# Placing the attention stages of a fused linear-attention and two-MoE kernel: scores one step later, decay and q scaling behind the hidden-layer work

## The reference

```python
for t in range(S):
    state = alpha[:, :, t, :, None] * state + np.einsum('bhd,bhe->bhde', k[:, :, t], v[:, :, t])
    y[:, :, t] = np.einsum('bhd,bhde->bhe', q[:, :, t], state)
# x = y as (B * S, H * D)
h = x @ w_in
x = (np.maximum(h, 0.0) + alpha * np.minimum(h, 0.0)) @ w_out
h = x @ w_in2
g = np.where(h >= 1, h, np.where(h <= -1, 0.0, (h + 1) ** 2 / 4))
y = g @ w_out2
```

## Time and profile before

| | us |
|---|---|
| median of 3 runs | 977.68 |
| lowest and highest | 975.34 and 981.53 |
| the profiled execution | 981.99 |
| its span | 980.3 |
| PE busy in it | 946.6 |
| DVE busy | 448.1 |
| ACT busy | 302.8 |
| POOL busy | 354.8 |
| mean granted clock of PE, share of full | 0.977 |

### The profile page before, as it was taken

How to read it: one execution, slowest core, us unless ns; L and a number is a source line. 1 busy time by engine, 2 the same in 40 slices (tenths; PEclk the granted TensorE clock), 3 DMA queues, 4 the chain that set the end, 5 groups by cost and what they waited for, 6 DMA issues and landing times.

```text
span 980.3 us, 13041 instructions
## 1 busy us (share of the span) xinstructions
PE 946.6 (97%) x5050; PEld 815.9 (83%) x5050; DVE 448.1 (46%) x732; ACT 302.8 (31%) x561; POOL 354.8 (36%) x322
## 2 busy tenths in 40 slices
PE   7888999899999999999999999999999999999998
PEld 6877999889988888888888888888888888888886
DVE  4566546656555554455532444333333333333332
ACT  2323222222322232232224543233233332332322
POOL 5234333323223232222324764434334334343332
PEclk8777999999999999999999999999999999999999
DMA  5721113111311111112011320010010010100101
GB/s 162 212 46 33 33 34 63 35 33 33 65 33 33 33 33 33 33 37 49 13 65 32 97 66 1 1 33 1 1 33 1 0 33 1 33 1 1 32 1 33
DMA packets 21101, 37.02 MB, mean 38 GB/s; under 512 B 2160, under 2 KB 14448, under 8 KB 21040
## 3 DMA queue, kind: packets, MB, share of 16 engines
q1 hardware_dynamic: 21040, 36.19, 15.7%
HBM read 31.47 MB, written 4.72 MB: 37 GB/s over the span
## 4 chain that ended last, share of the span: by engine, by line
issue 43%; PE 32%; POOL 20%; DVE 3%; DMA 1%; SPq 0%; ACT 0%; POOLq 0%; DVEq 0%; ACTq 0%
POOL g_lo L303 16%; PE h_ps L670 4%; PE y_ps L670 4%; PE y_ps L672 4%; PE y_ps L671 4%; PE h_ps L672 4%; PE h_ps L671 4%; PE a_ps L640 2%; POOL x_lo L310 2%; POOL w_lo L283 2%; PE a_ps L616 1%; PE a_ps L636 1%; PE a_ps L628 1%; DVE prod L467 1%; DVE inv L474 1%
## 5 line engine op out<-in xcount | busy, mean ns | idle before, releaser
L303 POOL TENSOR_TENSOR g_lo<-g,g_hi 128x512 fp32r<-128x512 f32 (+2 forms) x208 | 251.7, 1210 | 507.5 <-ACT g_hi L391 503.9
L384 ACT ACTIVATE g<-h_ps 128x512 f32<-128x512 f32 (+2 forms) x208 | 117.6, 565 | 493.9 <-PE h_ps L672 475.4
L670 PE MATMUL y_ps<-g_lo,w_hi 128*128 128x512 f32 (+2 forms) x624 | 234.4, 376 | 8.9 <-POOL g_lo L303 8.8
L670 PE MATMUL h_ps<-x_lo,w_hi 128*128 128x512 f32 (+2 forms) x624 | 240.9, 386 | 0.1
L672 PE MATMUL h_ps<-x_hi,w_lo 128*128 128x512 f32 (+2 forms) x624 | 234.2, 375 | 0.0
L671 PE MATMUL h_ps<-x_hi,w_hi 128*128 128x512 f32 (+2 forms) x624 | 233.9, 375 | 0.0
L672 PE MATMUL y_ps<-g_hi,w_lo 128*128 128x512 f32 (+2 forms) x624 | 233.3, 374 | 0.0
L671 PE MATMUL y_ps<-g_hi,w_hi 128*128 128x512 f32 (+2 forms) x624 | 233.3, 374 | 0.0
L531 DVE SCALAR_TENSOR_TENSOR g<-g 128x512 f32<-128x512 f32 x96 | 66.4, 692 | 248.7 <-ACT g L384 248.7
L670 PEld LDWEIGHTS y_ps<-g_lo,w_hi 128*128 128x128 f32 x624 | 118.2, 189 | 30.8 <-POOL g_lo L303 6.5
L524 DVE SCALAR_TENSOR_TENSOR g<-g,slopes,h_ps 128x512 f32<-128x512 f32 (+2 forms) x112 | 74.8, 669 | 142.9 <-ACT g L384 142.3
(11 more groups left out here) (69 smaller groups left out, 565.7 us busy)
## 6 DMA issues: line engine op xcount, KB each, us to landing
qka_sb<-qka SPq DMA_DIRECT2D x44, 288.0 KB, 4.8
y_all<-w SPq DMA_DIRECT2D x16, 384.0 KB, 6.4
qka_sb<-w SPq DMA_DIRECT2D x16, 384.0 KB, 3.1
v_sb<-v SPq DMA_DIRECT2D x24, 192.0 KB, 5.1
y<-y_all SPq DMA_DIRECT2D x18, 256.0 KB, 2.4
qka_sb<-qka SPq DMA_DIRECT2D x4, 192.0 KB, 4.2
qka_sb<-qka SPq DMA_DIRECT2D x4, 96.0 KB, 3.0
slopes<-slopes_in SPq DMA_DIRECT2D x1, 8.0 KB, 4.8
```

Of the source, the lines that this page charges most:

```text
L303: nc.gpsimd.tensor_tensor(g_lo[:, s % G_RING, 0:w_], g32[:, s % G32_RING, 0:w_], g_hi[:, s % G_RING, 0:w_].bitcast(F32), ALU.subtract).the ...
L384: nc.scalar.activation(g32[:, s % G32_RING, 0:w_], h_ps[s % 2][:, 0:w_], ACT.Relu, scale=-1.0 if first else 0.5, bias=0.0 if first else 0. ...
L670: nc.tensor.matmul(out_, wh, lo, start=start, stop=False)
```

## The change

Only the order changes; no instruction is added or removed. The lag of scores ahead of the turn goes from three steps to two, and that of decay from five to four. On POOL `hidden_lo` of s + 1 is issued ahead of `scale_q`. On DVE `decay` of a step is issued behind `activate(s + AHEAD)` of that step, ahead of the weight splits.

```diff
-        for _stage, _lag in (("decay", 5), ("scores", 3), ("mix", 1), ("turn", 0)):
+        for _stage, _lag in (("decay", 4), ("scores", 2), ("mix", 1), ("turn", 0)):
             PLAN.setdefault(_turn - _lag, []).append((_stage, _u))
...
+                    if s + 1 < STEPS:
+                        hidden_lo(s + 1)
                     for stage, u in plan_of(s):
                         if stage == "decay":
                             scale_q(u)
-                    if s + 1 < STEPS:
-                        hidden_lo(s + 1)
...
                         if stage == "mix":
                             update_state(u)
+                    activate(s + AHEAD)
+                    for stage, u in plan_of(s):
                         if stage == "decay":
                             decay(u)
-                    activate(s + AHEAD)
```

## The result

| us | before | after |
|---|---|---|
| median | 976.51 (4 runs, 974.12 to 981.53) | 1061.70 (4 runs, 1056.87 to 1062.27) |
| span of the profiled execution | 980.3 | 1060.5 |

The ratio is 1.0854, 95% interval 1.0799 to 1.0909: slower by 8.5%, 85 us. The forecast was 1054 us with a range of 1003 to 1090. The spans of the two profiled executions differ by 80.2 us, less than the medians, because the profiled execution before, 981.99 us, was over 4 us above its kernel's median.

What follows compares the result with a forecast made beforehand. TensorE (PE), busy 946.6 of 980.3 us, was taken as the bound. New stall 50.7, removed waits -14 and block 0 +3 gave +40; with clock +36, 977.7 + 76 = 1054 us, range 1003 to 1090.

Steps and rivals of the forecast that it cites:

- The new wait: PE stalls ahead of scores for the scaled k: 2.96 us per unit at 384, 2.5 at 512, 50.7 us in all.
- S: End of the first product of step t-2, which the activation ahead of decay needs; k was forecast relative to it.
- the unit at 113: Width-384 unit in the trace before, with decay directly behind an activation; model for k ready 7.65 us after that first product.
- Decay beside three POOL operations: Three POOL operations beside one decay, where the cycle at 418 had two, hold up DVE's scans and lengthen decay.
- Removed waits: Outside block 0, 10 PE waits for x_lo (6.7 us) and 6 for g_lo (4.1) go: -14 us with 3.2 extra.
- Without the clock: Whole kernel at unchanged clock: new stall 50.7, removed waits -14, block 0 +3, together +40 us.
- Clock, +36: PE's clock falls to half behind new waits: 12 falls in 19 units at 3.0 us each, bounds 0 and 57.
- Block 0, +3: Three units at width 256: one wait of about 5.4 us each replaces the old idle, +3 us, bounds 0 and +5.
- Rival 1: PE stalls for k outside and in block 0, but the clock holds: +40, 1018 us; chance 0.28.
- Rival 2: The stall for k is small, decay taking 5.6 to 5.9 us, and the clock holds: +17, 995 us; chance 0.09.
- rival 3: The scaled k isn't late for scores, so only the removed waits remain: faster, 961 us; chance 0.03.
- rival 4: Removed and added PE waits cancel, so the change does nothing: 978 us; chance 0.04.

Runs made afterwards that it cites:

- run 4: Changed kernel with the lags of before (decay 5, scores 3), both new orders kept: 1058.11 us, one run.
- run 5: Changed kernel with DVE's order undone (decay ahead of the activation again), lags and POOL's order as changed: 966.67 us, ratio 0.9910.
- run 6: Changed kernel with POOL's order undone (scale_q ahead of hidden_lo again), lags and DVE's order as changed: 1010.23 us, one run.
- run 7: Kernel before with the lags alone changed to 4 (decay) and 2 (scores), both orders as before: 966.33 us, ratio 0.9918.
- run 9: Kernel before with POOL's order alone changed (hidden_lo ahead of scale_q), lags 5 and 3: 972.77 us, ratio 0.9978.
- run 2: Changed kernel with 22, 13 and 9 small matmuls (widths 256, 384, 512) filling PE's wait for the scaled k: 1012.28 us, ratio 1.0369.
- run 10: Changed kernel with the lag of decay back at 5, scores at 2, both new orders kept: 973.11 us, ratio 0.9977.
- run 3: Changed kernel with 22, 7 and 4 small matmuls (widths 256, 384, 512) filling only part of PE's wait for k: 1018.74 us, ratio 1.0440.
- run 1: Changed kernel with 44, 26 and 18 small identity matmuls (widths 256, 384, 512) ahead of PE's wait for k: 1061.17 us, ratio 1.0879.

## Why the prediction was right

- **The new wait.** Right, to 0.15 us at 512 (S + 8.53 against 8.65) and to 0.4 at 384 (8.00 against 7.65, since prod and inv took 2.17 and 3.60 us where the unit at 113 had 1.83 and 3.25): the forecast was an idle time of 2.3 and 2.8 us, the trace shows 2.30 and 3.21. The step that carried it was to count PE's products between the point that releases decay and the point that needs k, and runs 4 and 5 bear it out: with both new orders 1058 to 1062 us at either pair of lags, with DVE's order undone 967.
- **Decay beside three POOL operations.** Right: prod 2.41 us, inv 3.64. Run 6 removes one of the three, and k comes 1.09 us sooner. I had weighed this as one term of a sum. It did more than that, because it took PE's wait at 512 from 1.5 or 1.8 us to 2.3, and behind the longer one the clock fell in 9 units of 12.
- **Removed waits**, taken at -14 us: those for x_lo and g_lo are gone. Their worth could not be seen in the changed kernel. Runs 7 and 5, where they are gone too outside block 0 but for small new ones (3 us in all in each), take 8.3 and 9.2 us less there than the kernel before, so -14 was somewhat high at most. One of the six waits for g_lo that the forecast removed, 0.53 us in the last step, behind all attention, stays. POOL's order by itself gives 3 us (run 9).
- **Without the clock** the forecast had 50.7 - 14 = +37 us outside block 0; run 2 shows +39.6.
- **Clock, +36**: the sum is close, its two factors are not. I took 12 falls in 19 units at 3.0 us each; there were 16, and they cost 40.2 us (run 2), 2.5 each, since five of them lasted only 3.4 us. That too few falls at too high a price made nearly the right product is luck, and 12 was a guess between bounds of 0 and 19.
- **Block 0, +3**: one wait of 5.28 to 5.52 us a unit, where I took 5.4; the stretch grew by 3.4 us. With the 2.9 us that the part ahead of it got shorter (13.7 us at half clock there in place of 20.2, which the change doesn't touch) the sum is 39.6 + 40.2 + 3.4 - 2.9 = 80 us, against 76.
- **Rivals.** Rival 1, that the clock holds, fell: 16 falls. Its price was near, though, since run 2 is that case outside block 0: +39.6 us there, and 1012 us in all against 1018. Rival 2 (waits near 1 us) and rivals 3 and 4 fell by the waits at L608. The rule of the Trainium skill that I set beside rival 1, in "TensorE: Matmul & The Clock Gate", section "Why this matters for your kernels", asks for no idle gaps over about 3 us. It would have kept full clock at 512, where the clock fell at 9 of 12 gaps of 2.3 us, so by this trace shorter gaps already matter; at 384 the gaps, 3.21 us, were longer than forecast and above it.

The lags, both in one move, are the good part of this change (run 7, -1%), POOL's order adds nothing to them (run 5), and DVE's order turns it into a loss: of 3.5% by itself (run 6), of 8.5% with POOL's beside it. Why single units at 2.3 us escape the fall and others don't was not settled, nor why the gaps of run 10 do.

## What to carry to other kernels

In an order written by hand, find for each long helper stage the event that releases it and the use that ends its slack, and count the work of the bounding engine between the two. "One step later" on both sides says nothing, if the release has moved behind an operation that itself waits for the bounding engine. And price a new wait twice: as idle time, and by what TensorE's clock does behind it. Here, ahead of light work, 2.3 us of wait cost about as much again in clock, and 1.5 us hardly anything, so a short filling, or a POOL operation moved out from beside a DVE scan, was worth up to 50 us.

## What the runs showed of the hardware

- Ahead of scores the clock fell at 3 of 19 single gaps of 1.4 to 1.7 us (run 3), 9 of 12 of 2.3 to 2.4 and 7 of 7 of 3.2 (changed kernel). Ahead of the first product of a block it fell at none of four, two of 2.23 and two of 3.09 us (run 10). After a fall outside block 0 it stayed at half for some 3 to 7 us.
- The light phases, scores and mix, with matmuls of 48 to 128 columns, did not let the clock fall by themselves: run 2 has the same ones at full clock from 29 us to 1008.
- An fp32 matmul of 128 columns on the identity is two instructions and takes 0.23 us in a row (4.18 us for 18, run 1), twice the 0.11 us that I had reckoned with.
